# TensorE multiplies a mask tile while VectorE solves the first tile and while the inverse travels

## The reference: what is computed

```python
k_n = k / (np.linalg.norm(k, axis=-1, keepdims=True) + 1e-06)
for t in range(S):
    kt, vt, bt = (k_n[:, :, t], v[:, :, t], beta[:, :, t, None])
    y[:, :, t] = np.einsum('bhd,bhde->bhe', q[:, :, t], state)
    v_old = np.einsum('bhde,bhd->bhe', state, kt)
    state = state + bt[:, :, :, None] * np.einsum('bhd,bhe->bhde', kt, vt - v_old)
x = relu(x @ w_in) ** 2 @ w_out
x = maximum(x @ w1, x @ w2, x @ w3) @ w_out2
```

## Time and profile before

| | us |
|---|---|
| median of 3 runs | 949.91 |
| lowest and highest of them | 947.35 and 950.4 |
| the profiled execution | 946.07 |
| its span | 944.1 |
| PE busy in the span | 868.9 (92%) |
| DVE, ACT, POOL busy | 428.9, 265.8, 285.4 |

### The profile page before, as it was taken

How to read it: one execution, slowest core, us unless ns; L and a number is a source line. 1 busy time by engine, 2 the same in 40 slices (tenths; PEclk the granted TensorE clock), 3 DMA queues, 4 the chain that set the end, 5 groups by cost and what they waited for, 6 DMA issues and landing times.

```text
span 944.1 us, 20905 instructions
## 1 busy us (share of the span) xinstructions
PE 868.9 (92%) x9148; PEld 743.6 (79%) x9148; DVE 428.9 (45%) x641; ACT 265.8 (28%) x464; POOL 285.4 (30%) x392
## 2 busy tenths in 40 slices
PE   2326699999999999999999999999999999999998
PEld 2326588878888888888888888887898989898988
DVE  6936365574566456645544444434323232323231
ACT  2211343233223322332233233633222222122221
POOL 4147898813941394139400000721000000000000
PEclk8658899999999999999999999999999999999999
DMA  7976764165424532353223134012020202010000
GB/s 185 220 142 148 160 148 102 52 138 132 106 60 97 131 105 60 93 129 80 64 63 91 36 95 123 9 51 67 1 67 1 67 1 67 0 67 1 34 1 34
DMA packets 123435, 76.27 MB, mean 81 GB/s; under 512 B 94320, under 2 KB 107120, under 8 KB 123344
## 3 DMA queue, kind: packets, MB, share of 16 engines
q1 hardware_dynamic: 121088, 73.89, 31.7%
q10 hardware_dynamic: 2256, 1.05, 0.4%
HBM read 53.18 MB, written 20.45 MB: 78 GB/s over the span
## 4 chain that ended last, share of the span: by engine, by line
PE 89%; DMA 3%; DVE 3%; SPq 3%; issue 1%; ACT 0%; ACTq 0%; DVEq 0%
PE psum L71 25%; PE psum L73 24%; PE psum L72 24%; PE psum L667 3%; PE psum L605 2%; PE psum L591 2%; PE psum L616 2%; PE psum L655 2%; PE psum L674 2%; PE psum L631 1%; PE psum L642 1%; DMA dram_f<-sol_f 1%; SPq L372 1%; DMA kz_first<-in_kT 1%; SPq L326 1%
## 5 line engine op out<-in xcount | busy, mean ns | idle before, releaser
L967 DVE TENSOR_TENSOR sq<-relu 128x512 f32<-128x512 f32 x96 | 76.2, 793 | 151.2 <-ACT relu L1103 151.1
L73 PE MATMUL psum<-x_lo,wb 128*128 128x512 f32 x324 | 126.3, 390 | 0.0
L72 PE MATMUL psum<-x_hi,wb 128*128 128x512 f32 x324 | 126.3, 390 | 0.0
L71 PE MATMUL psum<-x_hi,wb 128*128 128x512 f32 x324 | 126.2, 389 | 0.0
L71 PE MATMUL psum<-x_hi,win 128*128 128x512 f32 x288 | 116.3, 404 | 9.0 <-DVE x_lo L956 7.9
L1103 ACT ACTIVATE relu<-psum 128x512 f32<-128x512 f32 x96 | 57.3, 597 | 228.6 <-PE psum L73 228.6
L104 POOL TENSOR_TENSOR sol_tmp<-sol_b,sol_f 128x31 f32<-128x31 f32 (+15 forms) x155 | 90.1, 581 | 84.6 <-DMA sol_b<-dram_b 72.7
L71 PE MATMUL psum<-sq_hi,wout 128*128 128x512 f32 x288 | 114.2, 396 | 1.0 <-DVE sq_lo L972 1.0
L72 PE MATMUL psum<-x_hi,win 128*128 128x512 f32 x288 | 113.2, 393 | 0.0
L73 PE MATMUL psum<-x_lo,win 128*128 128x512 f32 x288 | 113.1, 393 | 0.0
L73 PE MATMUL psum<-sq_lo,wout 128*128 128x512 f32 x288 | 112.4, 390 | 0.0
(11 more groups left out here) (99 smaller groups left out, 1280.0 us busy)
## 6 DMA issues: line engine op xcount, KB each, us to landing
kz<-in_kT SPq DMA_DIRECT2D x40, 192.0 KB, 3.5
v_t<-in_vn SPq DMA_DIRECT2D x12, 384.0 KB, 3.5
qa<-in_qT SPq DMA_DIRECT2D x24, 192.0 KB, 3.8
nz<-in_kn SPq DMA_DIRECT2D x24, 192.0 KB, 4.3
x2T<-x SPq DMA_DIRECT2D x6, 768.0 KB, 4.1
x_raw<-x2T SPq DMA_DIRECT2D x6, 768.0 KB, 4.6
out_dram<-o_t SPq DMA_DIRECT2D x24, 192.0 KB, 1.9
raw_wb<-in_w SPq DMA_DIRECT2D x18, 192.0 KB, 4.4
```

The costliest lines, as they stand in the source:

```text
L71: nc.tensor.matmul(out, lhs_hi, rhs_hi, start=first, stop=False)
L72: nc.tensor.matmul(out, lhs_lo, rhs_hi, start=False, stop=False)
L73: return nc.tensor.matmul(out, lhs_hi, rhs_lo, start=False, stop=last)
L967: nc.vector.tensor_tensor(d.sq[:], d.relu[:], d.relu[:], ALU.mult).then_inc(s.sq_ready, 1)
```

## The change

Between `qk(0, 0)` and `x_block(0, 4)` in PE's program, 580 matmuls are put in. Each multiplies `mask` by `mask`, 128 partitions by 64 columns on both sides, and writes one of sixteen 64x64 places of bank 2. Nobody reads what they write. 300 of them are in 30 batches of ten, each batch behind a wait for four more steps of VectorE's solve; 280 follow without a wait.

```diff
+    SOLVE_LINKS = 4 * (HALF - 1) - 2
...
             qk(0, 0)
+
+
+            def idle_products(n):
+                for p in range(n):
+                    for h in range(2):
+                        nc.tensor.matmul(square_out(2, p % 8, h), d.mask[:], d.mask[:], start=True, stop=True)
+
+            pe.wait_ge(s.cg_ready, 2)
+            pe.wait_ge(s.mask_ready, 3)
+            for k in range(SOLVE_LINKS // 4):
+                pe.wait_ge(s.dve_link, 2 + 4 * (k + 1))
+                idle_products(5)
+            idle_products(140)
             x_block(0, 4)
```

## The result

The changed kernel takes 966.19 us (median of 4 runs, 964.0 to 967.11), the kernel before 950.15 us (4 runs, 947.35 to 952.12). The ratio is 1.0177, with a 95% interval of 1.0151 to 1.0204: the change costs 16 us. The forecast was +5.5 us, slower, with a range that ended at 960. The direction was right, and the size was wrong by a factor of three.

The account below looks back on a forecast made before the run. PE idles 27.7 us before x_block(0) and is the bound later on; instruction packets pace the products. E = 38.0 + 17.6 + 15.2 + 3.3 = 74.1, less 68.57 is +5.5; 949.91 + 5.5 = 955.4 us, range 949.5 to 960.

Parts of the forecast that it names:

- The products run in a row, and their waits do nothing: After qk(0): all 580 run one behind the other from 34.77 us, 58.75 ns each, 34.1 us in all.
- The rule of cost, E - 68.57: At x_block(0), begun by PE at E: the change costs E - 68.57 us, a difference that stays to the end.
- The instructions set the pace, one packet under way at a time: In the products: 2,320 added instructions, 254 records a packet, PE stops at packet ends; E from 71.1 to 80.1, 68%.
- the length of a round under full load: In the products until near 55 us: 4.4 us a round for four rounds, then 3.8 for four.
- the upper bound, 5.9 us a round: In the products' loaded rounds: 5.9 us each, from a packet begun 2.8 us after the end before it; E = 80.1.
- No stops: In the products: packets come ahead of PE, E = 68.85, +0.3 us, 950.2 us; chance 20%.
- Half clock: In the products: stops let the clock fall, 111 ns a product, E = 99.3, +30.7 us, 980.6 us; chance 3%.
- The clock falls later: At k_s(1): PE's wait grows from 2.08 to about 2.9 us, half clock costs 1.5 to 3 us more; 4% alone.
- Faster: At x_block(0): PE free by 62.5 and at full clock, 1.3 us won, 948.6 us; chance 5%.

Follow-up runs that it names:

- 79 wide, one half: Kernel before plus 79 matmuls of 512 columns, all writing the lower 64 partitions, no waits on the solve: 983.49 us, ratio 1.0369.
- 305 of 128 columns: Kernel before plus 305 matmuls of 128 columns, all writing the lower 64 partitions, no waits on the solve: 982.87 us, ratio 1.0357.
- products late: Changed kernel with 320 narrow products in a row, behind a wait for the stored inverse, in place of the 580: 963.29 us (one run).
- half of the products: Changed kernel with only the 300 products in the 30 batches, the 280 behind them left out: 949.57 us, ratio 1.0003.
- 79 wide, halves in turn: Kernel before plus 79 matmuls of 512 columns, writing upper and lower 64 partitions in turn, no waits on the solve: 948.2 us, ratio 0.9988.
- moved loads: Changed kernel with all 580 products, but weight pieces 1, 2 and 4 loaded only after the first inverse has come back: 973.64 us (one run).
- 60 products: Kernel before plus 60 matmuls of 512 columns, halves in turn: 949.79 us, ratio 1.0004; together with the moves 947.45 us, ratio 0.9977.
- the moves: Kernel before with ob and f1 of chunk 1 loaded earlier by SyncE and sums(2) before take_fd(0) on VectorE: alone 947.93 us, ratio 0.9976.
- 67 products: Kernel before with the moves and 67 matmuls of 512 columns: 947.31 us, ratio 0.9981.

## Why the prediction was right or wrong

**The products run in a row, and their waits do nothing: right.** They start at 36.83, at the end of `qk(0)`, in the middle of the solve. Two of the three stops lie behind the solve's end.

**The rule of cost, E - 68.57: right for large overruns.** E is the start of `x_block(0)`.

| kernel | E | by the rule | measured (difference of medians) |
|---|---|---|---|
| changed | 84.85 | +16.3 | +16.0 |
| 79 wide, one half | 103.31 | +34.7 | +34.5 |
| 305 of 128 columns | 103.52 | +35.0 | +33.9 |
| products late (one run) | 81.31 | +12.7 | +12.95 |
| half of the products | 69.28 | +0.7 | +0.6 |
| 79 wide, halves in turn | 71.37 | +2.8 | -1.5 |

For the last it is 4 us off. The profiled execution of before, from which 68.57 comes, was an early one: `qk(0)` started at 32.89 there and at 33.5 to 35.1 in the ten traces of the experiments, and without any overrun `x_block(0)` began at 65.09 and 65.42 in two of them, not at 62.64. So in a usual execution an overrun of 2 or 3 us is still free, and the rule says too much by that. In the changed kernel's trace losses further on make up for it. From `take_su(0)`, 16.67 us late, to the first `up` at 123.97, 19.67 us late (104.30 before), 3 us are added. Some 1.3 us are `k_s(1)` and `g_block(1)`, which ran at a clock of 0.50 (window of 102.0 to 105.4 above), 0.4 us a longer wait for instructions within `qk(1)`, and 1.3 us `y(1)`, here before and after:

```profile
94.33 2.09 PE L667 MATMUL psum<-qa,sw 128*64 128x64 f32 x64 [2.68 <-DVE sw L883]
...
112.75 3.39 PE L668 MATMUL psum<-qa,sw 128*64 128x64 f32 x64 [2.69 <-DVE sw L897]
```

Execution against execution, the changed kernel took 20.8 us more (966.88 for 946.07) and the rule gives 16.3. That it meets the difference of the medians, 16.0, is luck in part: two errors cancel.

**The instructions set the pace, one packet under way at a time: right.** The first stop came after 30 matmul records, which is the packet's end at 700 records that the count gave, and 81 packets were read. The later part, from 58.69 on, went at the forecast rate: 26.16 us for 6.83 packets, 3.83 each (forecast 3.8). As the forecast had packet and PE's own need (3.73) equally long there, this part does not tell the two apart.

**The failing step is the length of a round under full load**, "1.3 + 1.6 + 1.5 = 4.4 us a round". Measured were 8.66 and 7.85 us, and 9.49 and 8.66 with half of the products. Of the three terms the first one was wrong: from PE going on to the start of the next packet I took 1.3 us from a place at light load; under full load it was 5.4 to 6.8 us in these two kernels (and 4.1 and 4.7 us with the moved loads). Counted out, E came 10.75 us after the forecast 74.1: 2.1 from the later start of the products, 2.1 from the first stop (42.18 - 36.83 = 5.35 us from the start of the products to the second piece, 3.2 forecast), 6.6 from the rounds behind it (42.67 us against 36.1).

The sign had been in the trace. The one packet under full load, within 34.8 to 36.5, had come at least 2.8 us after its predecessor's end. I used it as the upper bound, 5.9 us a round, and took the value from the rows at light load because they had clearer times. Even the bound was too low, since that packet may have been asked for earlier than I counted. The range then cut off the slow end of that case.

**The rivals.** "No stops" fell, and with it the rule of the Trainium skill (page "Runtime: NRT & Kernel Launch", section "Instruction fetch mechanics") that crossing a block is mostly hidden: at a DMA share of 0.42 to 0.66 it was nearly so (one stop of 0.94 us over five packet ends), with the engines full it cost the changed kernel 2.4 to 4.3 us each time. "Half clock" was priced as all or nothing. It came in part: the two pieces behind the stops took 6.30 and 5.47 us instead of the 3.95 of the kernel with moved loads. So of the 13.9 us by which E lies behind 36.83 + 34.1, the stops are 9.0, the slow pieces 3.9, and a slightly slower pace (59.9 ns a product for 58.75) most of the rest. At full clock most of the 3.9 would have been waiting instead, as far as the two rounds of 7.30 and 7.29 us in the run with moved loads tell. "The clock falls later" happened: PE's wait ahead of `k_s(1)` was 3.13 us (forecast 2.9), and half clock cost 2.6 us of the 3 above (forecast 1.5 to 3). "Faster" was priced rightly in that there was almost nothing to collect.

## What to carry to other kernels

Work that is put in to fill an idle engine costs instructions as well as time; count them, and make them few and wide. 79 matmuls of 512 columns kept PE as busy as 580 of 64 did, for nothing instead of 16 us. A price must be taken from the row whose conditions are those of the new place (here the load on the DMA engines), not from the row with the sharpest times. And before a clock is kept up, ask what is late next: here it was a transfer behind others in a queue, and with that moved the products still added nothing that can be told.

## What the runs showed of the hardware

- Instruction packets share the DMA engines with the data. From PE going on to the next packet's start it took 1.3 us at a DMA share of 0.36 (changed kernel, from 58.69), 3.1 and 4.0 us at 0.92 and 0.96 (moved loads), and between 4.1 and 6.8 us at 1.04 to 1.11. What holds them there (a queue of descriptors, the order in which an engine serves its rings) no run shows, nor what spreads the last values.
- Float32 matmuls that write the lower and the upper 64 partitions in turn overlap: 79 products of 512 columns took 34.5 us so, and 68.0 us when all wrote the lower half.
- In the kernels with 60 products the clock fell while PE alternated between 1.2 us of work and 1.3 us of waiting, after a pause of 2.99 us (1.76 us with the moves); with 67 products and no such pause it held through the same steps and fell only in `k_s(1)`, behind a wait of 2.08 us.
